# Second MLP: the first product of a pair is copied from bank to bank, and the second is accumulated onto the copy

## What is computed

```python
def _moe2_ref(x, w_in, w_out) -> np.ndarray:
    h = x @ w_in            # 1536x512 by 512x2048
    g = h - np.tanh(h)
    return (g @ w_out).astype(np.float32)   # 2048x512
```

## Time and profile before

| what | value |
|---|---|
| median of 3 runs | 648.55 us (647.41 to 649.28) |
| the profiled execution, its own time | 645.95 us |
| its span | 644.2 us, so 1.75 us lie around it |
| TensorE matmuls busy | 626.1 us, 97% |
| VectorE, ScalarE, GpSimd busy | 384.7, 290.9, 121.1 us |
| granted TensorE clock | 1.0 of full speed (2.4 GHz) over the whole span |

### The profile page before, as it was taken

How to read it: one execution, slowest core, us unless ns; L and a number is a source line. 1 busy time by engine, 2 the same in 40 slices (tenths; PEclk the granted TensorE clock), 3 DMA queues, 4 the chain that set the end, 5 groups by cost and what they waited for, 6 DMA issues and landing times.

```text
span 644.2 us, 10662 instructions
## 1 busy us (share of the span) xinstructions
PE 626.1 (97%) x4086; PEld 584.6 (91%) x4086; DVE 384.7 (60%) x643; ACT 290.9 (45%) x564; POOL 121.1 (19%) x174
## 2 busy tenths in 40 slices
PE   8778999999999999999999999999999999999997
PEld 8568889999999998999889899999999989998886
DVE  2787577667753469766665555555433397666643
ACT  3675344444533247555554333333223275555542
POOL 3562712021210212222220000000100032222200
PEclk9999999999999999999999999999999999999999
DMA  9994913311312222322212421121313013322102
GB/s 259 207 203 122 207 51 91 91 41 51 91 51 60 63 91 69 95 66 66 66 50 66 147 62 55 56 62 48 99 50 113 2 51 89 88 68 67 33 2 98
DMA packets 101178, 53.91 MB, mean 84 GB/s; under 512 B 39880, under 2 KB 95176, under 8 KB 100936
## 3 DMA queue, kind: packets, MB, share of 16 engines
q1 hardware_dynamic: 99400, 50.08, 30.4%
q10 hardware_dynamic: 1728, 3.15, 1.3%
HBM read 50.07 MB, written 3.15 MB: 83 GB/s over the span
## 4 chain that ended last, share of the span: by engine, by line
PE 85%; SPq 6%; ACT 3%; DVE 3%; issue 1%; DMA 1%; POOL 0%; DVEq 0%; POOLq 0%; ACTq 0%
PE bank L714 14%; PE bank L715 14%; PE bank L716 14%; PE bank L822 7%; PE bank L821 7%; PE bank L820 7%; PE bank L774 6%; PE bank L778 6%; PE bank L776 6%; SPq L386 3%; PE bank L575 1%; PE bank L698 1%; SPq L343 1%; PE bank L678 1%; ACT kT L998 1%
## 5 line engine op out<-in xcount | busy, mean ns | idle before, releaser
L1396 DVE TENSOR_TENSOR h_lo<-pd,h_hi 128x384 fp32r<-128x384 f32 x112 | 66.1, 592 | 38.7 <-ACT h_hi L1078 24.5
L822 PE MATMUL bank<-y_hi,h_lo 128*128 128x512 f32 x192 | 75.5, 393 | 0.0
L821 PE MATMUL bank<-y_lo,h_hi 128*128 128x512 f32 x192 | 75.4, 393 | 0.0
L820 PE MATMUL bank<-y_hi,h_hi 128*128 128x512 f32 x192 | 75.3, 392 | 0.0
L561 POOL TENSOR_TENSOR ws_raw<-x_raw 128x256 f32<-128x256 f32 x16 | 12.0, 748 | 325.2 <-DMA x_raw<-in_moe_w_in_dram 145.4
L714 PE MATMUL bank<-xT_hi,x_hi 128*128 128x384 f32 x192 | 65.1, 339 | 1.5 <-DVE xT_lo L1392 1.5
L714 PE MATMUL bank<-xT_hi,y_hi 128*128 128x384 f32 x192 | 65.6, 342 | 0.0
L714 PE MATMUL bank<-h_hi,z_hi 128*128 128x384 f32 x192 | 64.9, 338 | 0.0
L716 PE MATMUL bank<-h_hi,z_lo 128*128 128x384 f32 x192 | 64.5, 336 | 0.0
L715 PE MATMUL bank<-h_lo,z_hi 128*128 128x384 f32 x192 | 64.5, 336 | 0.0
L716 PE MATMUL bank<-xT_hi,y_lo 128*128 128x384 f32 x192 | 64.3, 335 | 0.0
(11 more groups left out here) (139 smaller groups left out, 1443.3 us busy)
## 6 DMA issues: line engine op xcount, KB each, us to landing
x_raw<-in_moe_w_in_dram SPq DMA_DIRECT2D x32, 256.0 KB, 3.5
y_raw<-in_moe_w_out_dram SPq DMA_DIRECT2D x32, 256.0 KB, 2.8
x_raw<-in_moe_w_gate_dram SPq DMA_DIRECT2D x24, 256.0 KB, 3.1
y_raw<-in_moe_w_val_dram SPq DMA_DIRECT2D x24, 256.0 KB, 3.3
z_raw<-in_moe_w_out_dram SPq DMA_DIRECT2D x16, 384.0 KB, 3.3
qn<-in_q_dram SPq DMA_DIRECT2D x12, 256.0 KB, 6.4
out_dram<-stage ACTq DMA_DIRECT2D x12, 256.0 KB, 2.0
vw_early<-in_v_dram SPq DMA_DIRECT2D x12, 192.0 KB, 5.2
```

The costliest lines, as they stand in the source:

```text
L820: nc.tensor.matmul(AB[t][:], a_hi, w_hi, start=begins, stop=False, skip_group_check=True)
L821: nc.tensor.matmul(AB[t][:], a_hi, w_lo, start=False, stop=False, skip_group_check=True)
L822: last = nc.tensor.matmul(AB[t][:], a_lo, w_hi, start=False, stop=ends, skip_group_check=True)
L1396: nc.vector.tensor_tensor(dst, full, high.bitcast(f32), ALU.subtract).then_inc(done, 1)
```

## The change

ScalarE no longer copies P1 to SBUF but from `UB` to `VB`, and P2's six matmuls are issued without the start flag, so that they add onto the copy: `VB` then holds C11. VectorE's add for C11 goes; ScalarE's tanh and VectorE's subtraction read C11 from `VB`. TensorE's P2 now waits for the copy (`part_done`), and the next product in `VB` (P3 in the opening pair, P5 in the others) waits until VectorE has read C11 (`diff_done`) and no longer for the add (`total_done`). In ScalarE's `next_pair` the copy is put ahead of `split_sums`, which matters where i = 1. The diff, without its unchanged surroundings:

```diff
@@ -155,8 +155,8 @@
-            part = sb("part", [P, 3, NB], scope=second)
-            total = sb("total", [P, 3, NB], scope=second)
+            part = sb("part", [P, 2, NB], scope=second)
+            total = sb("total", [P, 2, NB], scope=second)
@@ -261,8 +261,8 @@
-        TOTALS0 = ("C11", "C12a", "C22", "C12")
-        TOTALS = ("C11", "C22", "C12")
+        TOTALS0 = ("C12a", "C22", "C12")
+        TOTALS = ("C22", "C12")
@@ -837,8 +837,8 @@  (TensorE, first_pair)
                 quarter(VB0, *operands(p, "P5"), start=True).then_inc(quarter_mm, 1)
-                quarter(VB, *operands(p, "P2"), start=True, rows=(0,))
                 pe.wait_ge(part_done, 3 * p + 1)
+                quarter(VB, *operands(p, "P2"), rows=(0,))
                 quarter(UB, *operands(p, "P6"), rows=(0,))
@@ -847,7 +847,7 @@
-                pe.wait_ge(total_done, total_no(p, "C11"))
+                pe.wait_ge(diff_done, tile_no(p, "C11"))
                 quarter(VB, *operands(p, "P3"), start=True).then_inc(quarter_mm, 1)
@@ -869,14 +869,13 @@  (TensorE, next_pair)
                 units(1 if i == 1 else 2)
-                pe.wait_ge(total_done, total_no(p - 1, "C12"))
-                quarter(VB, *operands(p, "P2"), start=True).then_inc(quarter_mm, 1)
+                pe.wait_ge(part_done, 3 * p + 1)
+                quarter(VB, *operands(p, "P2")).then_inc(quarter_mm, 1)
                 units(2)
                 pe.wait_ge(ws_lo_done, p + 1)
-                pe.wait_ge(part_done, 3 * p + 1)
                 quarter(UB, *operands(p, "P6")).then_inc(quarter_mm, 1)
                 units(2)
-                pe.wait_ge(total_done, total_no(p, "C11"))
+                pe.wait_ge(diff_done, tile_no(p, "C11"))
                 quarter(VB, *operands(p, "P5"), start=True).then_inc(quarter_mm, 1)
@@ -1106,15 +1105,24 @@  (ScalarE)
             def keep_part(p, k, product):
                 act.wait_ge(quarter_mm, quarter_no(p, product))
-                nc.scalar.copy(part[:, k, :], UB).then_inc(part_done, 1)
+                if k == 0:
+                    if p % NP:
+                        act.wait_ge(total_done, total_no(p - 1, "C12"))
+                    nc.scalar.copy(VB, UB).then_inc(part_done, 1)
+                else:
+                    nc.scalar.copy(part[:, k - 1, :], UB).then_inc(part_done, 1)
...
                     src = UB
+                elif name == "C11":
+                    act.wait_ge(quarter_mm, quarter_no(p, "P2"))
+                    src = VB
@@ -1143,9 +1151,9 @@  (ScalarE, next_pair)
                 tanh_tile(p - 1, "C12")
+                keep_part(p, 0, "P1")
                 if i == 1:
                     split_sums(p)
-                keep_part(p, 0, "P1")
@@ -1479,7 +1487,7 @@  (VectorE)
-                src = UB if name == "C21" else total[:, TOTALS.index(name), :]
+                src = {"C21": UB, "C11": VB}.get(name) if name in ("C21", "C11") else total[:, TOTALS.index(name), :]
@@ -1494,10 +1502,9 @@  (VectorE, first_pair)
-                add_total(p, "C11", "P2", 3 * p + 1, part[:, 0, :], VB)
```

More of the change, by code:

```diff
@@ L274, in total_no @@
         def total_no(p, name):
-            return 3 * p + (p + NP - 1) // NP + (TOTALS if p % NP else TOTALS0).index(name) + 1
+            return 2 * p + (p + NP - 1) // NP + (TOTALS if p % NP else TOTALS0).index(name) + 1
         def tile_no(p, name):
@@ L1496, in first_pair @@
                 x2_bottom(g, KC - 1)
-                add_total(p, "C11", "P2", 3 * p + 1, part[:, 0, :], VB)
-                add_total(p, "C12a", "P5", 3 * p + 2, part[:, 1, :], VB0)
+                add_total(p, "C12a", "P5", 3 * p + 2, part[:, 0, :], VB0)
                 diff_tile(p, "C11")
-                add_total(p, "C22", "P7", 3 * p + 3, part[:, 2, :], VB0)
+                add_total(p, "C22", "P7", 3 * p + 3, part[:, 1, :], VB0)
                 low_tile(p, "C11")
@@ L1531, in next_pair @@
                     split_z((g + 1) * ZG + 1)
-                add_total(p, "C22", "P5", 3 * p + 3, part[:, 2, :], VB)
+                add_total(p, "C22", "P5", 3 * p + 3, part[:, 1, :], VB)
                 diff_tile(p, "C22")
@@ L1535, in next_pair @@
                 low_tile(p, "C22")
-                add_total(p, "C12", "P3", 3 * p + 2, part[:, 1, :], VB)
+                add_total(p, "C12", "P3", 3 * p + 2, part[:, 0, :], VB)
                 low_tile(p, "C21")
```

## The result

The changed kernel takes 649.96 us (median of 20 runs, 648.64 to 651.83) against 648.24 us for the kernel before (20 runs, 646.01 to 650.83). The ratio is 1.0032 with a 95% interval of 1.0022 to 1.0042: slower, by about as little as can be told. The two medians lie 1.72 us apart, 0.27%, a little less than the ratio says. The time lies inside the predicted range. Of the three chances it was the one of 0.08 by the ratio, which is just above the limit of 0.3%; by the medians it would have been the one of 0.88. In the ratios further down, two executions that took 1585.74 us (before_again) and 1827.67 us (pool_late) are left out as slow.

The account below looks back on a forecast made before the run. TensorE was taken to bound the kernel, its matmuls busy 97% of the span. The only cost, 2 x 0.20 = 0.40 us from the second pairs, on the median of 648.55 gave 648.95 us; range 647.4 to 650.4.

Parts of the forecast that it names:

- TensorE bounds, and VectorE's adds are worth nothing: Second MLP: TensorE is the bound, so removing sixteen VectorE adds, 8.9 us of busy time, counts nothing.
- Later pairs: 0: Twelve pairs after the first two of each half: copy ends 0.34 us before P2 would lose time; cost 0.
- Opening pairs: up to 0.1 at P3, absorbed at P1: Two pairs, i = 0: P3 waits for C11's subtraction, 0.1 us at most, hidden by the next P1's wait; cost 0.
- The copy: 0.48, with 0.45 as the lower end: ScalarE's copy from bank to bank: taken as 0.48 us, like PSUM to SBUF, between 0.45 and 0.56.
- Second pairs, P2: 0.20: Two pairs, i = 1: one block doesn't cover the copy; P2 0.13 us late plus 0.07 of broken stream.
- Second pairs, P5: Two pairs, i = 1: C11's subtraction ends at 253.91, P5 could start at 254.06, due at 254.60; cost 0.
- The sum: Whole kernel: 2 x 0.20 = 0.40 us slower, all from the second pairs.
- Rival (a): Second pairs: reordered queues bring the sums' low part or C11's subtraction late, 0.2 to 0.4 us a half; 649.5; chance 0.17.
- (b): Later and opening pairs: each P2 loses 0.07 us though the copy is in time, 1.0 more; 649.9; chance 0.10.
- (c): Bank-to-bank copy much longer than 0.48 us, deciding at 0.82; 0.5 us longer gives 653.7; chance 0.05.
- The chances: Whole kernel: faster by over 0.3% 0.04, within 0.3% 0.88, slower by over 0.3% 0.08.

Follow-up runs that it names:

- before_again: The kernel before, unchanged, timed against itself: ratio 1.0013 [0.9996, 1.0030], 116.52 us a half of the second MLP.
- pool_late: Changed kernel, but GpSimd starts the third pair's weight sums only after C11's subtraction in the second pair: ratio 1.0043 against the kernel before, first half 117.99 us.
- p6_early: two_units, with P6 whole ahead of P2 and P2 whole ahead of P7 in the opening pair: ratio 0.9993 against the kernel before, 116.22 us a half.
- copy_thrice: Changed kernel with two extra ScalarE copies of P1 ahead of the bank copy in the twelve later pairs: 118.63 us a half, one run.
- diff_first: Changed kernel with C11's subtraction ahead of VectorE's x split in the second pair: ratio 1.0016 against the kernel before, 116.64 us a half.
- after_again: The changed kernel, unchanged, measured again: ratio 1.0022 [1.0009, 1.0036] against the kernel before, 117.13 us a half.
- two_units: diff_first, with two blocks between P1 and P2 and one between P2 and P6 in the second pair: ratio 0.9997 against the kernel before, 116.49 us a half.
- swap_back: Changed kernel with the cast of the weight sums ahead of the copy again in the second pair: 117.23 us a half, one run.
- before_p6: The kernel before, without the change, with only the opening-pair order of p6_early: ratio 0.9988 against the kernel before, 116.50 us a half.

## Why the prediction was right, and where it wasn't

- **TensorE bounds, and VectorE's adds are worth nothing.** Right as the kernel stood: no pair became shorter. p6_early shows the one exception, with another order.
- **Later pairs: 0.** Right, 92.54 for 92.53. The reckoned spare of 0.34 was somewhat too small: at P2 a release reaches the weight load in 0.05 us and not in 0.12 (changed kernel, copy_thrice), which leaves 0.43.
- **Opening pairs: up to 0.1 at P3, absorbed at P1.** Right: P3 starts at 247.56, 5.63 us after the first P1 where it was 5.64, its first matmul is stretched (0.42), and the pair takes 9.52 us.
- **The copy: 0.48, with 0.45 as the lower end.** It is 0.463 us in all sixteen, as the group shows:

```profile
L1114 ACT COPY bank<-bank x16: 463/463/463, 243.2 to 622.9; 128x384 f32<-128x384 f32 x16
```

  The Trainium skill, "ScalarE: Activation LUTs", Step-by-step: what each stage is for, calls PSUM ScalarE's faster target. The trace agrees: 0.463 to the bank, 0.480 to SBUF.
- **Second pairs, P2: 0.20.** Right in mechanism, 0.13 in size: 0.01 to 0.03 late for the 0.13 reckoned, and 0.10 to 0.11 of broken stream for 0.07. The prediction took both of its prices, 0.15 from release to matmul and 0.07 of stream, from P7 and P1. Those show them again in the changed kernel, but P2 and P5 show other ones, 0.05 and 0.10 to 0.11 (last section). The copy was also 0.02 shorter.
- **Second pairs, P5: "It moves by +0.67 for the sums and by about -0.48 for the add that is gone, to 253.35 ... Cost 0."** This is the step that failed. I moved VectorE's queue as a rigid row and asked only whether the subtraction itself would stretch beside GpSimd. It didn't (0.55 at 258.14, with one input in the bank). But the y split and the x split ahead of it read two SBUF tiles each, and the shift of 0.67 pushed the y split from before GpSimd's sums right into them. They took 1.23 and 1.22 for 0.68 and 0.77. That is 1.00 us, out of the 1.03 by which the subtraction came later than I had it (258.14 for 253.35 + 3.76 = 257.11). Its cover was 0.54. So P5 cost about 0.5 a half: the second pair is longer than diff_first's by 0.48 and 0.57 (15.07 for 14.59, 15.15 for 14.58), and by 0.50 and 0.49 in after_again. pool_late shows the stretch as the cause, diff_first and two_units that nothing else is behind it. The Trainium skill, "SBUF — State Buffer", Who interferes with whom, states that a VectorE instruction with one SBUF input doesn't contend with GpSimd, and that one with two contends with a GpSimd instruction that reads SBUF. The trace agrees: 0.55 with one, 1.23 and 1.22 with two.
- **The sum.** 0.40 forecast, 1.28 in the trace and 1.19 in its repeat: three times as much. That the time still lies inside the range owes more to the width of the range, 3.0 us for the spread of the medians, than to the sum; the median came out 1.0 above the forecast of 648.95. Rival (a), late queues at i = 1, is what happened, at about 0.5 a half on top, above its 0.2 to 0.4; it should have had more than 0.17, because the row of 1.09 in the earlier trace rows already showed a stretched neighbour. (b) and (c) didn't come: no gap at P2 in the later pairs.
- **The chances.** 0.08 for slower by over 0.3%. The trace's own 0.20% is within 0.3%, and the second measurement said 1.0022; that the first came out at 1.0032, just over the limit, may be the scatter ahead of the change, which isn't shown. So this chance is neither borne out nor refuted.

## What to carry to other kernels

When a step moves an engine's queue, move the queue and then ask for each instruction in it, not only for the last, what will now run beside it on GpSimd; a 0.7 us shift can cost another 1.0 us. Work taken from an engine that isn't the bound pays only where that engine's result is the next wait, so look for the order of work that makes it so (p6_early) before counting it. And if one operand of a chain goes to PSUM, count who must now have read it before the bank is free: here P5 had to wait for the end of the chain instead of its beginning.

## What the runs showed of the hardware

- A late release costs TensorE one of two amounts, and which one goes with the product. At P2 and P5 the weight load follows the end of the ScalarE or VectorE instruction by 0.05 us (258.69 to 258.74 after VectorE, 265.56 to 265.61 after ScalarE), the matmul is listed with 0.44 us, and the next one starts 0.27 to 0.29 later, for 0.18 in the stream. At P1 of the second pairs and P7 of the opening pairs in both kernels, at P3 of the opening pairs in the changed one, and at P4 of the second pairs in pool_late, the matmul follows the release by 0.15 (242.52 to 242.67 in the earlier trace rows, 261.26 to 261.41 in pool_late), is listed with 0.40 to 0.42, and the next one starts 0.24 to 0.26 later. In the program the first kind has one wait directly ahead of its matmuls and the second has two or more. Whether that makes the difference no run tests.
- The scatter ahead of the second MLP comes with waits of TensorE for the block sums from GpSimd, 0 (swap_back, with the earliest first P1) to 3.4 us (before_p6) in the thirteen profiles, and with its clock. What sets either isn't shown. In before_p6, which doesn't have the change, two stretches read (PE, PEld, DVE, ACT, POOL, clock, DMA share, GB/s):

```profile
78.00:82.00 4.00, 2.19 (x9) 1.50 (x10) 2.99 (x5) 2.50 (x5) 2.63 (x6) 0.70 1.16 222
...
82.00:86.00 4.00, 4.00 (x14) 3.91 (x14) 3.44 (x6) 0.51 (x1) 0.35 (x1) 0.50 0.10 21
```

  The matmuls were busy 2.19 of 4 us from 78 to 82, with a wait of 3.4 us around there, and the granted clock was 0.70 on the mean of that stretch and 0.50, which is 1.2 GHz, in the next. In the profile of the changed kernel the fall came later, 0.63 from 86 to 90, after 1.64 busy us of 4 from 82 to 86. In the first profile of the kernel before, the matmuls were busy 3.34 of 4 us from 78 to 82 and the clock stayed at 1.00.
